# Attention's first pairs: GpSimd's splits of heads 2 and 3, the order of SyncE's placements, and ScalarE's share of head 1

## The reference

```python
q_bits = einsum('bhsd,dk->bhsk', q, proj) > 0     # 6 bits a token, k alike
mask = q_bucket[:, :, :, None] == k_bucket[:, :, None, :]
scores = where(mask, (q @ k.T) / 8, -1e9); scores -= max(scores)
attn = exp(scores); attn /= sum(attn) + 1e-9; x = attn @ v
h = max(x @ w1, x @ w2, x @ w3); y = h @ w_out    # 1536 x 512, 768 wide
out = (h2 * sigmoid(1.702 * h2)) @ w_out2         # h2 = y @ w_in2, 2048 wide
```

## Time and profile before

| what | value |
|---|---|
| median of 3 runs | 682.2 us (680.92 to 682.27) |
| the profiled execution | 681.83 us, span 680.0 us |
| TensorE busy | 668.1 us, 98% |
| VectorE / GpSimd / ScalarE busy | 494.1 / 473.2 / 344.2 us |
| TensorE's mean granted clock | 0.995 |

### The profile page before, as it was taken

How to read it: one execution, slowest core, us unless ns; L and a number is a source line. 1 busy time by engine, 2 the same in 40 slices (tenths; PEclk the granted TensorE clock), 3 DMA queues, 4 the chain that set the end, 5 groups by cost and what they waited for, 6 DMA issues and landing times.

```text
span 680.0 us, 11978 instructions
## 1 busy us (share of the span) xinstructions
PE 668.1 (98%) x3902; PEld 578.7 (85%) x3902; DVE 494.1 (73%) x981; ACT 344.2 (51%) x756; POOL 473.2 (70%) x532
## 2 busy tenths in 40 slices
PE   8889999999999999999999999999999999999998
PEld 6766867777777689999999999988989989898986
DVE  6757788787888799878877953777777666555554
ACT  5757777778777741011102544455555555545433
POOL 4565647588886799987871618798888767777720
PEclk9889999999999999999999999999999999999999
DMA  6366548366253101211001200212222114221102
GB/s 153 81 155 163 136 109 187 90 160 149 71 146 122 33 0 32 63 32 32 23 24 48 83 12 31 63 62 63 81 77 92 63 55 164 62 63 62 37 27 93
DMA packets 58428, 54.36 MB, mean 80 GB/s; under 512 B 28640, under 2 KB 47232, under 8 KB 58368
## 3 DMA queue, kind: packets, MB, share of 16 engines
q1 hardware_dynamic: 56720, 53.21, 28.9%
q10 hardware_dynamic: 1648, 0.39, 0.3%
HBM read 32.51 MB, written 3.15 MB: 52 GB/s over the span
## 4 chain that ended last, share of the span: by engine, by line
PE 89%; POOL 5%; DVE 2%; ACT 1%; issue 1%; SPq 1%; DMA 1%; ACTq 0%; DVEq 0%; POOLq 0%
PE psO L1470 9%; PE psS L1448 9%; PE psR L1456 8%; PE psR L1518 7%; PE psR L1517 7%; PE psR L1519 7%; PE psS L1517 6%; PE psS L1519 6%; PE psS L1518 6%; PE psS L1618 4%; PE psS L1617 4%; PE psS L1616 4%; POOL w_lo L702 2%; PE psR L1396 1%; POOL w_raw L693 1%
## 5 line engine op out<-in xcount | busy, mean ns | idle before, releaser
L557 POOL TENSOR_SCALAR probs<-probs,lone,inv 128x768 f32<-128x768 f32 x96 | 94.0, 985 | 65.6 <-DVE inv L1081 65.6
L702 POOL TENSOR_TENSOR w_lo<-w_raw,w_hi 128x256 fp32r<-128x256 f32 x96 | 78.9, 835 | 45.6 <-ACT w_hi L921 44.8
L1063 DVE TENSOR_REDUCE neg_max<-psS 128x1 f32<-128x768 f32 x96 | 91.2, 950 | 16.3 <-PE psS L1448 12.2
L769 ACT ACTIVATE probs<-psS,neg_max 128x768 f32<-128x768 f32 x96 | 86.5, 901 | 22.6 <-DVE neg_max L1063 22.6
L540 POOL TENSOR_SCALAR w_hi<-w_raw 128x256 fp32r<-128x256 f32 (+1 forms) x79 | 49.2, 626 | 49.9 <-PE psS L1519 28.4
L1456 PE MATMUL psR<-ident,probs 128*128 128x128 f32 x576 | 74.9, 274 | 2.2 <-DVE w_hi L1053 1.3
L778 ACT ACTIVATE probs_t<-psR 128x384 f32<-128x384 f32 x128 | 59.5, 491 | 33.7 <-PE psR L1456 33.5
L1456 PEld LDWEIGHTS psR<-ident,probs 128*128 128x128 f32 x576 | 66.7, 141 | 6.7 <-issue 2.3
L1470 PE MATMUL psO<-probs_t,v_raw 128*64 128x384 f32 x384 | 69.8, 500 | 0.0
L1311 DVE TENSOR_TENSOR v_raw<-psR,early 128x384 f32<-128x384 f32 x64 | 35.4, 552 | 31.2 <-PE psR L1519 30.9
L1316 DVE TENSOR_TENSOR v_raw<-v_raw,bits 128x384 f32<-128x384 f32 x64 | 51.1, 799 | 7.9 <-ACT bits L944 5.5
(11 more groups left out here) (267 smaller groups left out, 1881.3 us busy)
## 6 DMA issues: line engine op xcount, KB each, us to landing
w_raw<-in_moe_w_in SPq DMA_DIRECT2D x16, 512.0 KB, 3.4
w_raw<-in_moe_w_out SPq DMA_DIRECT2D x32, 256.0 KB, 2.7
w_raw<-in_moe_w SPq DMA_DIRECT2D x9, 512.0 KB, 3.8
h_lo<-w_hi SPq DMA_DIRECT2D x22, 192.0 KB, 3.3
h_hi<-w_hi SPq DMA_DIRECT2D x18, 192.0 KB, 3.5
w_raw<-in_q SPq DMA_DIRECT2D x16, 192.0 KB, 3.3
v_raw<-in_v SPq DMA_DIRECT2D x16, 192.0 KB, 2.5
stacks<-w_hi SPq DMA_DIRECT2D x16, 192.0 KB, 3.3
```

The costliest lines, as they stand in the source:

```text
L557: pool.tensor_scalar(probs[i % PROBS][:, :], probs[i % PROBS][:, :], lone[:, i % 6:i % 6 + 1], inv[:, i % 6:i % 6 + 1], ALU.add, ALU.mult) ...
L702: pool.tensor_tensor(in2_slot(w_lo, n, which), in2_raw(n, PARTS2[which]), f32(in2_slot(w_hi, n, which)), ALU.subtract).then_inc(in2_split, 1)
L769: act.activation(probs[i % PROBS][:, :].rearrange("p (a b) -> p a b", a=2), psS[i % 2][:, :, 0:HALF], ACT.Exp, bias=neg_max[:, i % 6:i % 6 ...
L1063: dve.tensor_reduce(neg_max[:, i % 6:i % 6 + 1], psS[i % 2][:, :, 0:HALF], AX.XY, ALU.min).then_inc(max_ready, 1)
```

## The change

GpSimd makes head 2's high and low part between norm(2) and norm(3), head 3's high part behind norm(4), and head 3's low part between norm(5) and norm(6). SyncE sends head 2's marks behind head 3's high parts and ahead of its low parts. In head 1's own path ScalarE copies both turned halves and writes q's high part into `Q_LO` and `Q_HOT`; GpSimd starts there with the subtraction, and places three mark blocks, one of them q's; ScalarE places one; the DMA of q's high part goes. TensorE issues 9 more matmuls of zeros ahead of group 1.

```diff
--- before.py
+++ after.py
@@ -472,17 +472,15 @@
             load_qk(3)
             sync.wait_ge(dve_stacked, 4)
             sync.dma_start(f32(stack(1, K_HOT)[0:D, :]), f32(stack(1, K_LO)[D:P, :])).then_inc(first_placed, 16)
-            sync.wait_ge(pool_stacked, 4)
-            sync.dma_start(f32(stack(1, Q_HOT)[0:D, :]), f32(stack(1, Q_LO)[0:D, :])).then_inc(first_placed, 16)
             load_v(0)
             load_v(1)
             for p in range(1, PAIRS):
                 for m in (2 * p, 2 * p + 1):
                     if p + 1 < PAIRS:
                         load_qk(m + 2)
+                    place_hi(m)
                     if m == 3:
                         place_marks(2)
-                    place_hi(m)
                     place_lo(m)
                 for m in (2 * p, 2 * p + 1):
                     if m != 2:
@@ -605,44 +603,44 @@
                                    (t2, t3, hi11, ALU.add), (t2, t2, lo11, ALU.add))[step]
                 pool.tensor_tensor(o, one, two, op).then_inc(t_early, 1)
 
-            def first_q_hi(a):
-                pool.wait_ge(act_first, a + 1)
-                pool.wait_ge(dve_first, a + 1)
-                copy(stack(a, Q_LO)[0:D, :], qk_t[a][0:D, :]).then_inc(pool_stacked, 1)
-
-            def place_first(a, j):
+            def place_first(a, which, j):
 
                 pool.wait_ge(*emptied(("bits", 0, a)))
-                rows = 32 * (2 + j)
-                copy(half(stack(a, K_HOT)[D:D + MARKS, :], j), f32(first_marked[a][rows:rows + MARKS, :])).then_inc(pool_stacked, 1)
-
-            first_q_hi(0)
+                rows = 32 * (j + (2 if which == K_HOT else 0))
+                copy(half(stack(a, which)[D:D + MARKS, :], j), f32(first_marked[a][rows:rows + MARKS, :])).then_inc(pool_stacked, 1)
+
+            pool.wait_ge(act_first, 1)
+            pool.wait_ge(dve_first, 1)
+            copy(stack(0, Q_LO)[0:D, :], qk_t[0][0:D, :]).then_inc(pool_stacked, 1)
             pool.wait_ge(pool_stacked, 1)
             for j in range(2):
-                place_first(0, j)
+                place_first(0, K_HOT, j)
                 pool.wait_ge(pool_stacked, 2 + j)
-            first_q_hi(1)
-            pool.wait_ge(pool_stacked, 4)
+            pool.wait_ge(act_stacked, 5)
             pool.tensor_tensor(stack(1, Q_LO)[D:P, :], qk_t[1][0:D, :], f32(stack(1, Q_LO)[0:D, :]),
                                ALU.subtract).then_inc(pool_stacked, 1)
-            pool.wait_ge(pool_stacked, 5)
-            for j in range(2):
-                place_first(1, j)
-                pool.wait_ge(pool_stacked, 6 + j)
+            pool.wait_ge(pool_stacked, 4)
+            for n, (which, j) in enumerate(((K_HOT, 0), (K_HOT, 1), (Q_HOT, 1))):
+                place_first(1, which, j)
+                pool.wait_ge(pool_stacked, 5 + n)
             for n in range(GROUPS + 1):
                 p, st = n // 4, n % 4
                 if n > 0:
                     norm(3 * n - 1)
+
+                if n == 1:
+                    make_qk_hi(2)
+                    make_qk_lo(2)
+                if n == 2:
+                    make_qk_lo(3)
                 if n < GROUPS:
                     norm(3 * n)
                     norm(3 * n + 1)
+                    if n == 1:
+                        make_qk_hi(3)
                     if p > 0 and st < 2 and p + 1 < PAIRS:
                         make_qk_hi(2 * p + 2 + st)
                         make_qk_lo(2 * p + 2 + st)
-                    if n in (1, 3):
-                        make_qk_hi(2 + n // 2)
-                    if n in (2, 3):
-                        make_qk_lo(n)
                     if PAIRS // 2 <= p < PAIRS - 1 and st >= 2:
                         for step in range(6 * (p - PAIRS // 2) + 3 * st - 6, 6 * (p - PAIRS // 2) + 3 * st - 3):
                             if step < 16:
@@ -756,7 +754,7 @@
                 act.wait_ge(*filled(("turn", m, j)))
                 if m in (2, 3):
                     act.wait_ge(dve_stacked, (3, 5)[m - 2])
-                    act.wait_ge(pool_stacked, (1, 5)[m - 2])
+                    act.wait_ge(pool_stacked, (1, 4)[m - 2])
                 if m >= 4:
                     act.wait_ge(qk_lo_made, m - 3)
                 act.activation(half(qk_t[m % 2], j), bank(("turn", m, j))[:, 0:HALF], ACT.Copy,
@@ -783,14 +781,14 @@
                 act.wait_ge(unit_out, u + 1)
                 act.activation(x_hi[:, u // 2, ts(u % 2, HALF)], psO[:, 0:HALF], ACT.Copy).then_inc(x_hi_made, 1)
 
-            def first_copy_qk(a):
-                act.wait_ge(first_turned, 2 * a + 1)
-                act.activation(half(qk_t[a], 0), psS[a][:, 0, 0:HALF], ACT.Copy,
+            def first_copy_qk(a, j):
+                act.wait_ge(first_turned, 2 * a + j + 1)
+                act.activation(half(qk_t[a], j), psS[a][:, j, 0:HALF], ACT.Copy,
                                scale=qk_scale[:, 0:1]).then_inc(act_first, 1)
 
-            def first_hot(a, which, rows):
-                act.wait_ge(act_first, a + 1)
-                act.wait_ge(dve_first, a + 1)
+            def first_stack(a, which, rows):
+                act.wait_ge(act_first, 2 * a + 1)
+                act.wait_ge(dve_first, 1)
                 act.activation(stack(a, which)[0:D, :], qk_t[a][rows, :], ACT.Copy).then_inc(act_stacked, 1)
 
             def place_first(a, j):
@@ -804,12 +802,15 @@
             act.dma_start(qk_raw[1][:, :, 1, :], k_r[1, :, :, :]).then_inc(qk_loaded[1], 16)
             act.wait_ge(sides_set, 2)
             act.activation(table_probe[:, :], qk_scale[:, :], ACT.Exp)
-            first_copy_qk(0)
-            first_hot(0, Q_HOT, slice(0, D))
-            first_hot(0, K_HOT, slice(D, P))
+            first_copy_qk(0, 0)
+            first_stack(0, Q_HOT, slice(0, D))
+            first_stack(0, K_HOT, slice(D, P))
             for j in range(2):
                 place_first(0, j)
-            first_copy_qk(1)
+            for j in range(2):
+                first_copy_qk(1, j)
+            first_stack(1, Q_LO, slice(0, D))
+            first_stack(1, Q_HOT, slice(0, D))
             for n in range(GROUPS + 1):
                 p, st = n // 4, n % 4
                 if n > 0:
@@ -817,8 +818,7 @@
                 if n < GROUPS:
                     exp_tile(3 * n)
                 if n == 0:
-                    for j in range(2):
-                        place_first(1, j)
+                    place_first(1, 0)
                 if n > 0:
                     copy_turned(3 * n - 2, 0)
                 if n < GROUPS:
@@ -1045,7 +1045,7 @@
             def make_bits(p):
                 dve.wait_ge(*filled(("bits", p)))
                 if p == 1:
-                    dve.wait_ge(act_stacked, 6)
+                    dve.wait_ge(act_stacked, 7)
                     dve.wait_ge(pool_stacked, 7)
                 else:
                     for a in range(2):
@@ -1120,20 +1120,17 @@
                 dve.tensor_scalar(proj_block[rows, first:first + NBITS], proj_raw[:, :], sign, None,
                                   ALU.mult).then_inc(proj_signed, 1)
 
-            def first_copy_qk(a):
-                dve.wait_ge(first_turned, 2 * a + 2)
-                dve.wait_ge(sides_set, 2)
-                dve.tensor_scalar(half(qk_t[a], 1), psS[a][:, 1, 0:HALF], qk_scale[:, 0:1], None, ALU.mult).then_inc(dve_first, 1)
-
             def first_k_hi(a):
-                dve.wait_ge(act_first, a + 1)
-                dve.wait_ge(dve_first, a + 1)
+                dve.wait_ge(act_first, 2 * a + 1)
+                dve.wait_ge(dve_first, 1)
                 dve.tensor_copy(stack(a, K_LO)[D:P, :], qk_t[a][D:P, :]).then_inc(dve_stacked, 1)
 
             def halves(x):
                 return x.rearrange("p (j s) -> p j s", j=2)
 
-            first_copy_qk(0)
+            dve.wait_ge(first_turned, 2)
+            dve.wait_ge(sides_set, 2)
+            dve.tensor_scalar(half(qk_t[0], 1), psS[0][:, 1, 0:HALF], qk_scale[:, 0:1], None, ALU.mult).then_inc(dve_first, 1)
             first_k_hi(0)
             dve.wait_ge(marks_made, 10)
             make_first_bits(0)
@@ -1405,8 +1401,8 @@
 
             def first_project(a):
 
-                pe.wait_ge(act_first, a + 1)
-                pe.wait_ge(dve_first, a + 1)
+                pe.wait_ge(act_first, 2 * a + 1)
+                pe.wait_ge(dve_first, 1)
                 pe.wait_ge(proj_signed, 4)
                 o = ring_bank(("bits", 0, a))
                 for g in range(4):
@@ -1433,9 +1429,9 @@
                 if i >= 2:
                     pe.wait_ge(probs_ready, i - 1)
                 if n < 2 and t == 0:
-                    pe.wait_ge(act_stacked, (4, 6)[a])
+                    pe.wait_ge(act_stacked, (4, 7)[a])
                     if a == 1:
-                        pe.wait_ge(first_placed, 32)
+                        pe.wait_ge(first_placed, 16)
                     pe.wait_ge(dve_stacked, (3, 5)[a])
                     pe.wait_ge(pool_stacked, (3, 7)[a])
```

(2 more changed lines are left out.)

## The result

Over 8 runs of each, the changed kernel has a median of 677.64 us (676.75 to 679.32) and the kernel before 681.36 (680.02 to 682.27): 3.7 us less, ratio 0.9947 with a 95% interval of 0.9934 to 0.9961. The profiled execution took 677.34 us with a span of 675.5, 4.5 less than the one profiled before.

The account below looks back on a forecast made before the run. TensorE, busy in 98% of the span, was taken as the bound, with time to win only before about 50 us. 4.67 + 0.9 = 5.6 us off gave 676.2 for the profiled execution, forecast 676.4, range 674.9 to 679.2.

Parts of the forecast that it names:

- (a): Start: the clock falls all the same and GpSimd's lateness eats the rest; 4.3 to 4.7 us off, 677.7; chance 0.14.
- the larger term: Tile 12's scores: the wait for head 2's marks and the half clock behind it go, 4.67 us.
- the smaller one: Groups 0 to 2: earlier first tiles and a clock that stays up, 0.9 us.
- The stall of tile 12: Head 2's late marks at tile 12: 2.81 us of waiting and 1.86 of half clock, 4.67 us gone.
- The start: Groups 0 to 2: 0.3 to 0.5 us from head 1's path, 0.7 from the clock, less GpSimd's lateness; 0.9 taken.
- I take 0.9: Tile 9's and tile 12's scores come 0.7 to 1.0 us earlier; 0.9 taken, bounds -0.4 and 1.4.
- slack of six microseconds: Head 3's low part, made by 31 and issued at 33, is wanted only at tile 15, six microseconds on.
- the rival of a slowed GpSimd: Groups 1 to 3: GpSimd's splits slowed by 1.66 beside VectorE, 3.0 us late; 684.2 us; chance 0.05.
- (b): Tile 12: marks still late, one microsecond of stall left and the clock falling; 2.7 us off, 679.5; chance 0.10.
- (c): Nothing measurable: another DMA in the same queue, the low parts' landing, is just as late; about 682 us; chance 0.04.
- (d): Groups 1 to 3: slower, GpSimd becomes the bound; 6.7 us lost at the start against 4.67 won; 684.2; chance 0.05.
- the sum: Whole kernel: 4.67 + 0.9 = 5.6 us off the profiled execution's 681.83, giving 676.2.

Follow-up runs that it names:

- the run with head 2's parts alone: Kernel before, with only head 2's high and low part moved between norm(2) and norm(3): 680.95 us, 0.7 below, ratio 0.9986.
- the edit that frees the flag: Changed kernel with VectorE's flags of tiles 6 and 7 made one column at a time: 676.55 us, ratio 0.9921 to the kernel before.
- The two edits that avoid the overlap: Changed kernel, either with flags of tiles 6 and 7 made one column at a time (676.55 us) or head 3's low part behind norm(7) (676.85 us).
- the splits alone: Kernel before with only the change's moved splits of heads 2 and 3 and its SyncE order: 677.5 us, 3.9 below, ratio 0.9944.
- the version with 18: Changed kernel with head 3's low part behind norm(7), bits before inverse sums, 18 matmuls of zeros for 9: 675.97 us, ratio 0.9919.

## Why the prediction was right, and the step that failed

The measured 677.64 lies in the stated range, but its gain of 3.7 lies below the 4.8 to 6.5 that the forecast itself stood for, and nearest to the number of rival (a), whose cause did not occur in the profiled execution. So the larger term was right, the smaller one failed, and that the range held owes something to its width.

The stall of tile 12: right, in mechanism and size. SyncE had been behind head 2's low parts; made between norm(2) and norm(3), they leave it free, the marks go out with their bits, and 4.68 us go against 4.67 forecast, the half-clock stretch among them. SyncE's timetable was a microsecond too short (the low parts' issues ended at 25.15 and not at 24, since the four issues of the high parts stand ahead of them; head 3's high parts ended at 29.49 and not at 28.5), still before the bits at 30.58. That head 3's early splits belonged to it I had put down as slack of six microseconds; the run with head 2's parts alone shows them to be needed.

The start: the step "I take 0.9" failed. It measured 0.13. Up to tile 6's scores the forecast held: 23.29 against 23.95, so 1.1 us won once the later beginning of this execution (0.47) is taken off; but of that, head 1's path gave only 0.16 at tile 3's scores (0.5 forecast; the third placement ended at 16.33, and the scores start 0.14 behind it, which I had left out), and the rest is the clock that stayed up: tile 4's scores took 0.94.

GpSimd's lateness at norm(3) and norm(4) took 0.6 back at tile 7 (25.57 against 25.65). Then the price of head 3's low part was mis-sized: I counted 0.35 for GpSimd's own lateness and asked of the port rule only what it does to the placements. Its price was 1.45 us (1.62 against 0.17) of VectorE's time on the way to the bits. TensorE's wait for them grew by 0.57 over the kernel before, and the edit that frees the flag takes 0.85 off it. Tile 9's scores start at 31.00 against 30.50: with the 0.47 taken off, the whole 1.1 is gone. The two edits that avoid the overlap have medians 0.8 and 1.1 us below the change's.

What I had set against the rival of a slowed GpSimd was that its split at 31.48 ran its 1.82 "with VectorE's minima and small operations beside it". The row was true and did not bear on the question: GpSimd was not the engine that is held, and the small flags beside it were 128x1. In the profile before, 17 of the 32 flags of 128x2 took 0.30 to 0.55 instead of 0.17, and each of them ended within 0.04 us of the end of a GpSimd instruction, be it a scaling, a copy or an operation on two tiles; this should have been looked up. The Trainium skill states the rule in full (SBUF — State Buffer, "SBUF: two separate sides"): a VectorE operation in a two-port performance mode also contends for the shared pair, and the loser waits for the whole instruction. The Trainium skill's page VectorE: DVE Perf Modes ("What auto-detection actually checks") says that, where firmware enables it for the instruction, the engine takes a two-port mode by itself if a single source and the destination lie in SBUF and their outermost sizes above one are both even or equal. The runs agree: in eight places of seven kernels a 128x2 flag was held by a low part for 1.22 to 1.72 us, each to within 0.03 us of its end, and the 128x1 form never. It is not the column count alone: VectorE's reciprocal on 128x2 ran in its 0.17 inside GpSimd's subtraction of head 2 (22.32, in the profile of the change). That the mode is the reason was not measured; no run changes it alone.

Rivals: (a), a clock that falls all the same, may be what one in eight runs of the change shows (0.994); where it fell in that run isn't seen. (b) and (c) did not occur. (d), GpSimd as the bound of the first groups, was near in its place but not in its way: VectorE was held for GpSimd, not GpSimd slowed, and no clock fell behind it in the profiled execution, though it did in that of the splits alone, behind 1.96 us of idle time.

The profiled execution took 677.34, 1.1 above the 676.2 that the sum gives for it: 0.77 is the start, 0.47 the later beginning, and somewhat over 0.1 came back behind tile 15. The median of 677.64 is 1.2 above the forecast of 676.4. The gain was 5.6 by the forecast's sum and 3.7 by the medians; what the start doesn't explain of it is mostly the profiled execution of before, which lay 0.47 above its kernel's median over eight runs and on which the sum was built.

## What to carry to other kernels

Idle time of one engine is not free time if another shares its access to memory: before moving work into it, list what the other engine issues in that stretch, the smallest instructions too, and ask what stands behind them in its list. A stall that goes brings the next deadline forward by as much, so look at the next transfer of the same kind before counting the gain. A short stretch of idle matmuls in front of a known wait cost nothing here, and the version with 18 kept its clock in all six runs; that they were the cause is not shown. Where single executions begin up to 0.9 us apart, compare profiles from the first moment that the change can't have touched.

## What the runs showed of the hardware

VectorE's `tensor_scalar` on 2 numbers a partition took 1.22 to 1.72 us beside a GpSimd subtraction of 1.82, and ended with it; on 1 number a partition it took 0.14 beside the same subtraction, and a reciprocal on 2 numbers took its 0.17. The mean granted clock differs from run to run of one kernel: 1.000 or 0.999, 0.997 with one stretch at half clock, 0.995 or 0.994 with two. Without the 9 matmuls the step from 1.000 to 0.994 was worth 2.2 us, so about 1.1 for each of two such stretches, an estimate from the profiles of other kernels with that mean clock, and less than the 1.86 that I had put on one. Waits of 1.2 to 1.7 us in front of tile 3 were followed by a stretch at half clock in four profiles and by none in seven.
